# Contracting 64 rows in every matmul: two chunks' products in the two halves of TensorE's array

## The reference

```python
w = exp(weight_gen - max_k(weight_gen)); w = w / (sum_k(w) + 1e-9)      # (4, 4096, 8 heads, 7 taps)
out[b, s, h, g] = sum_k w[b, s, h, k] * x_pad[b, s + k, h, g]           # causal window of 7 tokens, 6 rows of zeros ahead
h = out.reshape(16384, 192) @ w_in                                      # 192 -> 2048
g = where(h > 0, h, exp(min(h, 0)) - 1)                                 # ELU
return g @ w_out                                                        # 2048 -> 192
```

## Time and profile before

| what | value |
|---|---|
| runs | 1204.04 us (1203.97 to 1204.1) |
| profiled execution | 1204.23 us, of which the span of the core 1202.4 us |
| TensorE matmuls busy | 1183.3 us, 98% (6683) |
| weight loads busy | 1071.6 us, 89% |
| ACT, POOL, DVE busy | 957.5, 779.2 and 767.7 us (80%, 65%, 64%) |
| granted TensorE clock | 0.998 of full speed |

### The profile page before, as it was taken

How to read it: one execution, slowest core, us unless ns; L and a number is a source line. 1 busy time by engine, 2 the same in 40 slices (tenths; PEclk the granted TensorE clock), 3 DMA queues, 4 the chain that set the end, 5 groups by cost and what they waited for, 6 DMA issues and landing times.

```text
span 1202.4 us, 19288 instructions
## 1 busy us (share of the span) xinstructions
PE 1183.3 (98%) x6683; PEld 1071.6 (89%) x6683; DVE 767.7 (64%) x1309; ACT 957.5 (80%) x1786; POOL 779.2 (65%) x359
## 2 busy tenths in 40 slices
PE   5999999999999999999999999999999999999998
PEld 4899999999999999999999999999999999999997
DVE  6666666666656666666666566666666665666655
ACT  5888787887887887878878878878788788788786
POOL 7966785556865567765568655678555686555700
PEclk9999999999999999999999999999999999999999
DMA  7122221222111222112221112221122211221000
GB/s 236 34 81 81 65 67 31 80 81 80 52 51 58 80 80 64 66 31 80 81 80 52 51 58 80 80 64 67 31 80 80 81 51 42 67 80 44 27 31 14
DMA packets 51919, 79.37 MB, mean 66 GB/s; under 512 B 5416, under 2 KB 34852, under 8 KB 51872
## 3 DMA queue, kind: packets, MB, share of 16 engines
q1 hardware_dynamic: 51872, 78.90, 21.5%
HBM read 54.50 MB, written 24.38 MB: 66 GB/s over the span
## 4 chain that ended last, share of the span: by engine, by line
PE 96%; POOL 3%; DMA 0%; issue 0%; DVE 0%; SPq 0%; ACT 0%; DVEq 0%; POOLq 0%
PE slot L859 49%; PE acc L870 29%; PE acc L874 17%; POOL prod L436 1%; POOL prod L444 1%; DMA xwin<-in_x_dram 0%; POOL wout L481 0%; POOL prod L452 0%; POOL prod L453 0%; POOL win_lo L481 0%; POOL win_rest_lo L481 0%; POOL first_mixed L464 0%; POOL first_rest L465 0%; DVE outs L790 0%; PE slot L846 0%
## 5 line engine op out<-in xcount | busy, mean ns | idle before, releaser
L808 DVE SCALAR_TENSOR_TENSOR slot<-em,slot 128x512 f32<-128x512 f32 x512 | 356.3, 696 | 411.6 <-ACT em L655 406.2
L870 PE MATMUL acc<-wout,g_hi 128*128 128x384 f32 x2048 | 461.8, 338 | 0.5 <-DVE g_lo L814 0.5
L649 ACT ACTIVATE em<-slot 128x512 f32<-128x512 f32 x512 | 305.2, 596 | 187.9 <-PE slot L859 187.8
L870 PEld LDWEIGHTS acc<-wout,g_hi 128*128 128x128 f32 x2048 | 372.7, 188 | 43.0 <-issue 1.2
L814 DVE TENSOR_TENSOR g_lo<-slot,g_hi 128x512 fp32r<-128x512 f32 x511 | 349.4, 684 | 0.1
L655 ACT ACTIVATE em<-em 128x512 f32<-128x512 f32 x512 | 323.5, 632 | 16.3
L874 PE MATMUL acc<-wout,g_lo 128*128 128x192 f32 x2048 | 326.0, 266 | 0.0
L874 PEld LDWEIGHTS acc<-wout,g_lo 128*128 128x128 f32 x2048 | 311.2, 190 | 2.4
L436 POOL TENSOR_TENSOR prod<-xwin,probs 128x5376 f32<-128x5376 f32 (+1 forms) x33 | 306.6, 9294 | 6.4 <-POOL xt L473 5.2
L662 ACT ACTIVATE g_hi<-slot 128x512 fp32r<-128x512 f32 x511 | 297.1, 582 | 0.1
L859 PE MATMUL slot<-xt,win_hi 128*128 128x512 f32 (+1 forms) x515 | 215.0, 418 | 1.5 <-ACT xt L582 1.5
(11 more groups left out here) (70 smaller groups left out, 535.0 us busy)
## 6 DMA issues: line engine op xcount, KB each, us to landing
xwin<-in_x_dram SPq DMA_DIRECT2D x29, 960.0 KB, 5.1
out_dram<-outs SPq DMA_DIRECT2D x32, 384.0 KB, 2.6
turned_dram<-turned SPq DMA_DIRECT2D x120, 96.0 KB, 2.0
x_main<-turned_dram SPq DMA_DIRECT2D x30, 256.0 KB, 2.9
x_rest<-turned_dram SPq DMA_DIRECT2D x60, 128.0 KB, 3.0
wg<-in_weight_gen_dram SPq DMA_DIRECT2D x32, 112.0 KB, 2.5
xwin<-in_x_dram SPq DMA_DIRECT2D x2, 768.0 KB, 4.4
wout_raw<-in_moe_w_out_dram SPq DMA_DIRECT2D x4, 384.0 KB, 8.9
```

What stands on the lines that cost most here:

```text
L649: nc.scalar.activation(em[:, i % 2, :], slot[s][:], ACT.Exp).then_inc(s_exp, 1)
L808: nc.vector.scalar_tensor_tensor(out=slot[s][:], in0=em[:, i % 2, :], scalar=0.0, in1=slot[s][:], op0=ALU.min, op1=ALU.max).then_inc(s_g, 1)
L870: pe.matmul(acc[j][:, 0:2 * d_model], g_hi[:, f % GBUFS, chunk(j)], wout[:, f, :], start=(f == 0), stop=False)
```

## The change

Every matmul of the steady part contracts 64 rows and uses one half of the partitions. Matmuls come as couples, one with rows 0 to 63 and one with rows 64 to 127, each with its own weights and its own PSUM bank.

- First products (`half_products`): the 192 input features are three pieces of 64. x is held twice, in both halves. The lower half holds the weights of chunk 2m, the upper those of chunk 2m + 1 (`win_hi`, `win_lo` in a new layout, loaded in pieces of 128 columns). Nine couples (high x high, low x high, high x low, for three pieces) make both chunks' products in two banks.
- Second products (`second_products`): a chunk's 128 features are two halves, both needed by every token tile. In step j the lower half's features go to tile j and the upper half's to tile j + 2 (mod 4). A step has four couples: high and high of both chunks, low and low of both. So that the two halves never write one bank at a time, a step waits until the step before last has ended (`s_row`).
- Order: TensorE makes the first products of pair m + 1, then the second products of pair m.
- ELU: for the even chunk as before. For the odd chunk ACT makes only the exp; DVE subtracts one and takes min(., 0) in place in `em` with a tensor_scalar, then takes the max with the bank.
- Around it: the high and low parts of x are three of 128x512 each in place of two; the high parts stand behind pairs 4, 5 and 6 (one each), POOL's low parts behind the window products in place of ahead of them. Block 1 goes through DRAM as the others do. The weights' low parts of block 0 are made by DVE alone, after the first three with both inputs in SBUF. `mixed` is made by one addition in place of two.

The diff, cut to its core:

```diff
+    PIECES = d_model // REST
+    PASSES = 3 * PIECES
+    assert PIECES * REST == d_model and CHUNKS % (2 * PAIR) == 0
+
+    def slot_of(f):
+        return (PAIR + f) % SLOTS
...
-                        sp.wait_ge(s_xtlo, b.count(2, -4))
-                    sp.dma_start(x_main[:], turned_dram[q, 0:P, :]).then_inc(s_back, 16)
+                    sp.wait_ge(s_gone, b.count(16 * QUADS))
...
-                    main, rest = first_mixed[:, q, first_tile:, :], first_rest[:, q, first_tile:, :]
...
+                    for h in range(2):
+                        last = nc.gpsimd.tensor_tensor(first_mixed[:, first_tile * PIECES:, h, :], one, two, ALU.add)
                 else:
-                    main, rest = mixed[:, q, :, 0:P], mixed[:, q, :, P:]
...
-                nc.gpsimd.tensor_tensor(rest, one[:, :, P:], two[:, :, P:], ALU.add).then_inc(s_add, 1)
+                    one, two = (t.rearrange("p (t d) -> p t d", d=d_model) for t in (one, two))
+                    last = nc.gpsimd.tensor_tensor(mixed[:, q, :, :], one, two, ALU.add)
...
+            def exponential(b, f):
+
+                act.wait_ge(s_filled, b.count(CHUNKS, f + 1))
+                ge(act, s_g, b.count(CHUNKS, f - 1))
+                nc.scalar.activation(em[:, f % 2, :], slot[slot_of(f)], ACT.Exp).then_inc(s_exp, 1)
...
+            def high(b, f):
+
+                act.wait_ge(s_g, b.count(CHUNKS, f + 1))
+                ge(act, s_row, used_count(b, f - GBUFS))
+                nc.scalar.activation(g_hi[:, f % GBUFS, :], slot[slot_of(f)], ACT.Copy).then_inc(s_ghi, 1)
...
             def body(b):
...
-                        act.wait_ge(s_filled, ring_count(b, pos))
-                        ge(act, s_g, b.count(CHUNKS, i - 1))
-                        nc.scalar.activation(em[:, i % 2, :], slot[s][:], ACT.Exp).then_inc(s_exp, 1)
...
-                        act.wait_ge(s_exp, b.count(CHUNKS, i + 1))
-                        nc.scalar.activation(em[:, i % 2, :], em[:, i % 2, :], ACT.Copy,
-                                             bias=-1.0).then_inc(s_em, 1)
...
+                for m in range(CHUNKS // 2):
+                    one, two = 2 * m, 2 * m + 1
+                    exponential(b, one)
+                    act.wait_ge(s_exp, b.count(CHUNKS, one + 1))
+                    nc.scalar.activation(em[:, 0, :], em[:, 0, :], ACT.Copy, bias=-1.0).then_inc(s_em, 1)
+                    exponential(b, two)
+                    high(b, one)
+                    if m == 0 and b.has_previous:
+                        cross_terms(b, 1)
+                    high(b, two)
+                    if b.first and m in SPLIT_AT:
+                        hi_half(*SPLIT_AT[m])
+                    if m == softmax_at(b)[1] and b.has_after_next:
...
+                    if b.has_next:
+                        at = turn_at(b)[1]
+                        if b.first and m == at:
+                            high_parts(b, range(PIECES))
+                        elif not b.first and at <= m < at + PIECES:
+                            high_parts(b, (m - at,))
...
+            def low_half(kind, a):
+
+                n = SPLITS.index((kind, a))
+                hi, lo, raw = split_of(kind, a)
...
+                else:
+                    dve.wait_ge(s_whi, n + 1)
+                    nc.vector.tensor_tensor(lo, raw, hi.bitcast(F32), ALU.subtract).then_inc(s_wlo, 1)
...
-                for j in range(TILES):
+                for j, t in enumerate(DONE):
                     dve.wait_ge(s_cross, b.count(TILES, j + 1 - n_before * TILES))
-                    nc.vector.tensor_tensor(outs[:, parity, j, :], acc[j][:, 0:d_model], cross[:, j, :],
+                    nc.vector.tensor_tensor(outs[:, parity, t, :], acc[t][:, 0:d_model], cross[:, t, :],
                                             ALU.add).then_inc(s_out, 1)
...
+            def low(b, f):
+
+                dve.wait_ge(s_ghi, b.count(CHUNKS, f + 1))
+                nc.vector.tensor_tensor(g_lo[:, f % GBUFS, :], slot[slot_of(f)], g_hi[:, f % GBUFS, :].bitcast(F32),
+                                        ALU.subtract).then_inc(s_split, 1)
+
             def body(b):
...
-                        dve.wait_ge(s_em, b.count(CHUNKS, i + 1))
-                        nc.vector.scalar_tensor_tensor(out=slot[s][:], in0=em[:, i % 2, :], scalar=0.0,
-                                                       in1=slot[s][:], op0=ALU.min, op1=ALU.max).then_inc(s_g, 1)
...
+                for m in range(CHUNKS // 2):
+                    one, two = 2 * m, 2 * m + 1
+                    dve.wait_ge(s_em, b.count(CHUNKS // 2, m + 1))
+                    nc.vector.scalar_tensor_tensor(out=slot[slot_of(one)], in0=em[:, 0, :], scalar=0.0,
+                                                   in1=slot[slot_of(one)], op0=ALU.min, op1=ALU.max).then_inc(s_g, 1)
+                    dve.wait_ge(s_exp, b.count(CHUNKS, two + 1))
+                    nc.vector.tensor_scalar(em[:, 1, :], em[:, 1, :], -1.0, 0.0, op0=ALU.add,
+                                            op1=ALU.min).then_inc(s_emlow, 1)
+                    dve.wait_ge(s_emlow, b.count(CHUNKS // 2, m + 1))
+                    nc.vector.tensor_tensor(slot[slot_of(two)], em[:, 1, :], slot[slot_of(two)],
+                                            ALU.max).then_inc(s_g, 1)
+                    if m == 0 and b.has_previous:
 
                         dve.wait_ge(s_stored[1 - q], b.per_parity(16, 16 * q))
                         outputs(b, 1, 1 - q)
...
+                    low(b, one)
+                    low(b, two)
+                    if b.first and m in SPLIT_AT:
+                        low_half(*SPLIT_AT[m])
...
-            def one_pass(parity, f, s, k, tokens=slice(0, N)):
-
-                cols = chunk(f)
-                w, v = ((win_hi[:, cols], xt[:, parity, 0, tokens]), (win_lo[:, cols], xt[:, parity, 0, tokens]),
-                        (win_hi[:, cols], xt_lo[:, parity, tokens]), (win_rest_hi[:, cols], xt[:, parity, 1, tokens]),
-                        (win_rest_lo[:, cols], xt[:, parity, 1, tokens]))[k]
-                return pe.matmul(slot[s][:, tokens], w, v, start=(k == 0), stop=(k == PASSES - 1))
...
-                    pe.wait_ge(s_ghi, b.count(CHUNKS, f + 1))
-                    for j in range(TILES):
-                        hi(j)
-                    pe.wait_ge(s_split, b.count(CHUNKS, f + 1))
-                    for j in range(TILES):
-                        last = lo(j)
-                    last.then_inc(s_used, 1)
...
+            HALVES = (slice(0, REST), slice(REST, P))
+
+            def half_products(parity, m, passes, tokens=slice(0, N)):
+
+                cols = chunk(m)
+                for n in passes:
+                    k = n % PIECES
+                    w, v = ((win_hi, xt), (win_lo, xt), (win_hi, xt_lo))[n // PIECES]
+                    for h, rows in enumerate(HALVES):
+                        last = pe.matmul(slot[slot_of(2 * m + h)][:, tokens], w[rows, k, cols],
+                                         v[rows, parity, k, tokens], start=(n == 0), stop=(n == PASSES - 1))
+                        if n == PASSES - 1 and tokens.stop == N:
+                            last.then_inc(s_filled, 1)
+
+            def second_products(b, m):
+
+                one, two = 2 * m, 2 * m + 1
+                hi = (g_hi, slice(0, 2 * d_model))
+                lo = (g_lo, slice(d_model, 2 * d_model))
+                pe.wait_ge(s_ghi, b.count(CHUNKS, two + 1))
+                for j in range(TILES):
+                    if m == 0 and j < 2:
+
+                        ge(pe, s_out, b.count(TILES, 2 * j + 2 - TILES))
+
+                    ge(pe, s_row, b.count(STEPS, 2 * TILES * m + 2 * j - 2))
+                    for n, (f, (g, cols)) in enumerate(((one, hi), (two, hi), (one, lo), (two, lo))):
+                        if j == 0 and n == 2:
+                            pe.wait_ge(s_split, b.count(CHUNKS, two + 1))
+                        for h, rows in enumerate(HALVES):
+                            t = (j + 2 * h) % TILES
+                            last = pe.matmul(acc[t][:, cols], g[rows, f % GBUFS, chunk(t)],
+                                             wout[rows, f, 0:cols.stop - cols.start],
+                                             start=(f == 0 and n == 0 and j < 2),
+                                             stop=(f == CHUNKS - 1 and n == 3 and j >= 2))
+                            if n == 3:
+                                last.then_inc(s_row, 1)
...
+                for m in range(CHUNKS // 2):
+                    n = m + 1
+                    if n < CHUNKS // 2:
+                        if not (b.first and n < 2):
+                            ge(pe, s_split, b.count(CHUNKS, 2 * (n - 1)))
+                            if b.first and n % 2 == 0:
+                                pe.wait_ge(s_wlo, SPLITS.index(("in", n // 2)) + 1)
+                            half_products(q, n, range(PASSES))
...
```

(6 more changed lines are left out.)

435 lines of the change are left out of this document (136 added, 299 removed).

## The result

The changed kernel takes 1677.22 us (1676.79 to 1677.98, 4 runs); the kernel before takes 1204.07 us (1203.97 to 1204.1) beside it. The ratio is 1.3929, 95% interval 1.3912 to 1.3946: 473 us slower. The forecast was 1172 us and its range ended at 1590; even the rival that had the cause, the port (1575), was 102 us short.

A forecast was written before the change was run, and what follows sets the result against it. TensorE's own program was taken as the bound (96% of the chain of waits). 1204.2 - 66.6 (couples) + 31 (boundary) + 4 (start) = 1172.6, forecast 1172 us; range 1130 to 1590, likeliest case 1135 to 1205.

The forecast's parts named there:

- the port: Rival: DVE's SBUF-only tensor_scalar waits for POOL's whole operations, +13 us a block, 403 in all, 1575 us; chance 0.20.
- the price of the tensor_scalar: DVE's new step in the pair's chain takes t = 0.42 us, so low parts come at 4.56, needed at 4.69.
- The couples: On TensorE, two 64-row matmuls run at the price of one: 4.34 us a pair against 4.60, -66.6 us.
- The row waits: TensorE's wait before each group of eight matmuls on an earlier group's end: taken as zero, 31 us at worst.
- The chain with t = 0.68: Through ACT and DVE, a tensor_scalar of 0.68 us makes the low parts 0.13 us late per pair, +33 us.
- The boundary: At a block's end TensorE waits 1.0 us for low parts behind copies and outputs, 31 times: +31 us.
- The fetch of x: x fetched back in both halves, 768 KB for 512, has 10 us before it is asked for; no cost.
- The start: Prologue: transposes and weight loads for both halves, block 0's weight low parts on DVE: +4 us (0 to +12).

The follow-up runs named there:

- e1: Changed kernel with the odd chunk's DVE tensor_scalar replaced by a scalar_tensor_tensor with a second input in PSUM, and the following max taking over min(., 0): 1314.28 us.
- e7: e6 with the -1 of both chunks on ACT, in the order exp, exp, -1, -1, high, high, and no tensor_scalar on DVE: 1204.58 us.
- e9: e7 with x's fetch, softmax steps and high parts moved in blocks 0 and 1, and the high parts made in one go there: 1191.47 us.
- e6: e5 with the block boundary's cross copies and outputs split in two parts, the high and low parts between them: 1232.29 us.
- e5: e1 with the turn on DVE, which starts the fetch of x, one pair earlier in every block but the first: 1237.81 us.
- e4: e1 with the first products' couples taken apart, nine passes of the lower half and then nine of the upper: 1419.46 us.

## Why the prediction was wrong

**The step that failed** is the price of the tensor_scalar: "With t = 0.42, between them, the chain ends at 4.56", which put the wait for POOL at nothing and left it to a rival with a chance of 0.20. What the runs show in its place is a mean of 1.96 us, with 93 of 256 held to the end of a POOL operation, and 363 us for it in all. 0.42 came out right to the digit for an undisturbed instruction (816.45); that is luck, since it was chosen between 0.18 and 0.68 from no row of its kind. The two rows that decide were both there: a subtract with two SBUF inputs stretched past POOL's op, and the DVE steps of the ELU with an operand in PSUM that are not stretched. The argument against, "it has one SBUF input, not two", rested on no row.

The Trainium skill (SBUF — State Buffer, Who interferes with whom) states the exclusion for DVE in a two-port mode and names tensor_scalar among the operations that can enter one. The 9.22 us beside POOL's 9.70 agree; in which mode it ran no trace shows. A rule of the Trainium skill with a stretched row beside it deserved more than half of the weight.

One sentence of the prediction is wrong besides: not all steady DVE ops had an operand in PSUM. The softmax maximum of the earlier trace rows, a tensor_reduce from SBUF to SBUF, took its 0.38 us at 618.50 inside this POOL operation of the kernel before. So SBUF operands alone don't make an instruction wait:

```profile
617.23 1.85 POOL L453 TENSOR_TENSOR prod<-prod 128x768 f32<-128x768 f32 x1
```

**The rival's size.** It had 13 us a block, 403 in all, for what gets past the slack. The tensor_scalars are longer by 502.4 - 256 x 0.42 = 394.9 us, and TensorE waits 363.7 us ahead of its second products where it waits 78.0 in e1: 286 us more. The spans of the two differ by 366.8, so some 81 us are left for the slower clock (0.865 for 0.975; after a wait 0.70 us a group for 0.37) and whatever else differs. The port with its clock thus cost 363 us, less than the rival's 403. It was 102 us short because of the other terms, 142 us between the forecast and e1, which it had taken over from the forecast.

**The couples: right,** in mechanism and size. 4.34 us a pair was forecast, 4.36 measured in e7 and e9. The row waits cost at most those 0.02, so the zero for them holds.

**The chain with t = 0.68: right in size.** The text had 0.13 us for every pair, +33 us. In e6 it is 0.31 for three of a block's eight pairs, and taking the step off DVE (e7, which changes ACT's order too) gave 27.7.

**The boundary: right in size, half in mechanism.** 1.0 us a block forecast; the pair at the boundary takes 0.9 us more than 4.36 in e1, 1.2 in e5, 1.0 in e6 and 1.1 in e7. The forecast had one wait, for the low parts; in e7 that one is 0.77 us and a second, at the outputs, 0.33.

**The fetch of x: wrong.** "It has 10 us before it is asked for", at no cost. It had 8.4 and needs 10.6, and cost 76.5 us in e1. Its time could have been estimated from before's trace, where pieces of 128 and 256 KB took 3.0 and 2.9 us from issue to landing (the two of 384 KB take 4.8); the text named the larger size and didn't price it.

**The start: wrong in size.** +4 (0 to 12) forecast, about 26 in e7. At least two of the port's cases are in it, and the DRAM round trip of block 1, which had no term of its own.

The terms put together: forecast 1172.6, + 33 (t = 0.68) + 76.5 (fetch) + 22 (start) + 5 (256 x 0.02) + 4 (boundary) = 1313, and e1, the change without the port's waits, took 1314.3. This is bookkeeping and proves no single term: the fetch was measured as a difference from e1 itself, and the start is what e7's steady blocks leave over. From there to 1677.2 is the port with the clock that falls behind it, 363 us. How these 363 split between the stall, the clock and a fetch that the stalls cover (ACT's wait for x is 6.8 us in the changed kernel, 62.6 in e1) isn't separated by a run. Nor was a kernel made that takes out the rest of the start (some 13 us) or the boundary's 35. These two, with the couples' gain of (4.60 - 4.36) x 256 = 61 us, are why e9 is 13 us faster and not 60.

## What to carry to other kernels

Before an elementwise step moves to DVE while POOL has long operations, look at its kind and at where its operands live. A tensor_scalar from SBUF to SBUF, and a tensor_tensor with both inputs in SBUF, waited here for the rest of the POOL operation in flight, up to 9.9 us, with a slower clock behind the wait; a tensor_reduce in SBUF didn't. The form with an operand in PSUM took the price away at 0.26 us an instruction. Treat a new round trip or a larger transfer as a term with its own duration against its own lead, and the first two blocks apart from the steady ones. Half-row matmuls on separate halves did run at the price of one, loads too, so that repacking a contraction that full rows fill badly (192 in 128s) gained nearly what the count says in the steady pairs (61 of 66.6 us); whether any of it is left depends on the waits around it.

## What the runs showed that was not expected

- Weight loads of the two halves start 3 to 4 ns apart; 108 to 111 ns still lie between two loads of one half. A couple of 192 columns goes every 0.09 to 0.11 us.
- The starts on TensorE's two halves don't follow the order of the program strictly: in e4 the upper half ran three to four matmuls ahead of its place.
- A tensor_tensor with two SBUF inputs is stretched by POOL as regularly as the tensor_scalar: in e7 it ends 0.81 to 0.83 us after POOL's operation, where alone it takes 0.96. The 128x512 ops with an operand in PSUM took 0.67 to 0.70 us at all times.
